# Weight operands split straight into the slot of a pair, their stores moved, attention blocks respaced

## The reference

```
attn:  q, k, v of (4, 8, 576, 64), cut into chunks of 64 rows;
       softmax(q_c k_c^T / 8) v_c inside each chunk  ->  x of 2304 tokens x 512
mlp 1: h = x @ w_in (512 x 2048);  g = h - tanh(h);               x = g @ w_out (2048 x 512)
mlp 2: h = x @ w_in (512 x 2048);  g = h * tanh(log(1 + exp(h))); out = g @ w_out
```

## Time and profile before

| | |
|---|---|
| device time, median of 2 | 1030.31 us (1028.92 to 1031.69) |
| the profiled execution, its device time | 1033.9 us |
| span from its first to its last instruction | 1032.1 us |
| PE busy | 860.1 us, 83% |
| DVE, ACT, POOL busy | 609.7, 381.0, 228.2 us |
| mean granted clock of TensorE | 0.907 |
| DMA | 180.48 MB, mean 175 GB/s |

### The profile page before, as it was taken

The page is one execution under the profiler, slowest core; times in us unless marked ns, Lnnn a source line. Parts: engine busy times, 40 slices in busy tenths (PEclk is TensorE's granted clock), DMA queues, the critical chain, the costliest instruction groups (busy, mean ns, idle before and its releaser), DMA issues.

```text
span 1032.1 us, 13626 instructions
## 1 busy us (share of the span) xinstructions
PE 860.1 (83%) x5298; PEld 782.0 (76%) x5298; DVE 609.7 (59%) x871; ACT 381.0 (37%) x539; POOL 228.2 (22%) x325
## 2 busy tenths in 40 slices
PE   8978667498547677998767666999999999999998
PEld 7977666498546566887666666898898988898986
DVE  6754445276324444663454443788888777787776
ACT  4432332142222222432233323455455344454453
POOL 4221433331222333323453432011110000000000
PEclk9988878799878788998888887999999999999999
DMA  7542456622435554444556587345396133752211
GB/s 249 180 137 89 144 165 220 209 79 104 171 147 181 203 200 167 153 154 174 203 214 214 214 318 273 119 157 198 140 385 234 74 143 120 309 204 102 113 72 62
DMA packets 51456, 180.48 MB, mean 175 GB/s; under 512 B 8768, under 2 KB 12608, under 8 KB 51392
## 3 DMA queue, kind: packets, MB, share of 16 engines
q1 hardware_dynamic: 33696, 112.74, 30.1%
q0 software_dynamic: 17696, 66.86, 18.4%
HBM read 125.04 MB, written 50.59 MB: 170 GB/s over the span
## 4 chain that ended last, share of the span: by engine, by line
PE 45%; DMA 10%; DVE 6%; POOL 4%; ACT 3%; issue 1%; ACTq 0%; DVEq 0%
PE psum L1473 6%; PE psum L1474 6%; PE psum L1472 6%; PE psum L1454 6%; PE psum L1455 6%; PE psum L1453 6%; DMA t_lo<-o_lo 5%; DMA s_lo<-o_lo 4%; DVE o_lo L934 2%; ACT o_hi L656 2%; PE psum L1337 2%; PE psum L1356 1%; PE psum L1338 1%; PE psum L1339 1%; PE psum L1357 1%
## 5 line engine op out<-in xcount | busy, mean ns | idle before, releaser
L934 DVE TENSOR_TENSOR o_lo<-pool_words,o_hi 128x768 fp32r<-128x768 f32 (+1 forms) x54 | 47.0, 870 | 116.2 <-ACT o_hi L656 116.2
L1454 PE MATMUL psum<-w_lo,w_hi 128*128 128x384 f32 x288 | 97.6, 339 | 0.0
L656 ACT ACTIVATE o_hi<-pool_words 128x768 fp32r<-128x768 f32 (+1 forms) x54 | 41.7, 772 | 150.9 <-DMA t_lo<-o_lo 74.0
L1455 PE MATMUL psum<-w_hi,w_lo 128*128 128x384 f32 x288 | 97.0, 337 | 0.0
L1453 PE MATMUL psum<-w_hi 128*128 128x384 f32 x288 | 96.3, 335 | 0.7 <-DVE pool_words L1111 0.7
L1337 PE MATMUL psum<-x_hi,w_hi 128*128 128x384 f32 x32 | 17.5, 548 | 94.0 <-DVE pool_words L1005 93.9
L1278 PE MATMUL psum<-g_hi,w_hi 128*128 128x384 f32 x128 | 50.1, 391 | 44.2 <-DMA pool_words<-pool_words 44.2
L1337 PEld LDWEIGHTS psum<-x_hi,w_hi 128*128 128x128 f32 x32 | 9.2, 286 | 96.8 <-issue 96.8
L1337 PE MATMUL psum<-w_hi 128*128 128x384 f32 x192 | 66.5, 346 | 15.4 <-DVE pool_words L994 13.1
L1474 PE MATMUL psum<-w_hi,g_lo 128*128 128x512 f32 x192 | 76.1, 396 | 0.0
L1473 PE MATMUL psum<-w_lo,g_hi 128*128 128x512 f32 x192 | 75.9, 395 | 0.0
(11 more groups left out here) (171 smaller groups left out, 2395.3 us busy)
## 6 DMA issues: line engine op xcount, KB each, us to landing
w_hi<-s_hi SPq DMA_DIRECT2D x40, 896.0 KB, 5.5
w_lo<-s_lo SPq DMA_DIRECT2D x40, 896.0 KB, 7.8
pool_words<-w POOLq DMA_DIRECT2D x32, 256.0 KB, 3.7
pool_words<-w_out POOLq DMA_DIRECT2D x32, 256.0 KB, 5.5
t_hi<-o_hi POOLq DMA_DIRECT2D x21, 384.0 KB, 3.5
t_lo<-o_lo POOLq DMA_DIRECT2D x21, 384.0 KB, 5.3
w_hi<-t_hi SPq DMA_DIRECT2D x18, 384.0 KB, 5.5
w_lo<-t_lo SPq DMA_DIRECT2D x18, 384.0 KB, 7.3
```

What stands on the lines that cost most here:

```text
L656: act.activation(step_halves(k)[0], step_source(k), ACT.Copy).then_inc(step_hi_done, 1)
L934: dve.tensor_tensor(lo, step_source(k), hi.bitcast(f32), ALU.subtract).then_inc(step_lo_done, 1)
L1454: pe.matmul(ps, a_hi, t_lo_words[:, k, :], start=False, stop=False, skip_group_check=i in (M5, M3))
L1455: mm = pe.matmul(ps, a_lo, t_hi_words[:, k, :], start=False, stop=end, skip_group_check=i in (M5, M3))
```

## The change

1. Weight operands of `w1` ("direct" steps) are split straight into the slot of their pair: no buffer, no store before use, and no `load_slot` for the first wide group. PE's `product1` waits for the split's parts. `keep_slot`, by SP, writes a finished slot to DRAM for the second wide group; `load_slot` is left for pairs 8 to 15 and the second MLP.
2. The other steps are spread anew: w2's operands 0 and 1, w1's 0 and 1 and two token steps in group 1 of the plain stage (none in group 0), w1's 2 to 7 beside pairs 1 to 6, w2's 2 to 7 beside pairs 8 to 14, the second token set beside pairs 9 to 15.
3. From w2's operand 3 on, `STEP_BUFFER` alternates between buffer 0 and a new buffer 2 (the second weight step stays in 1), and a third raw buffer holds every other operand.
4. Steps of pair 8 and later are stored by SP (`by_sync`), the rest by POOL; on POOL the stores now stand ahead of the sums.
5. Blocks 3 to 11 are respaced; `keep_x(t)` waits for `shift(t + 1)` and stands behind the exp; `shift` no longer waits for `keep_x`.
6. Two of the four last `y1` steps of the plain groups move ahead of pair 0; three token-operand splits (`x1_hi`, `x1_lo`) and block 12's normalisation move with them.

```diff
-TOKEN_STEPS = (M1, M5, M3, M7, M6, M2, M4)
+TOKEN_STEPS = (M1, M2, M5, M3, M7, M6, M4)
-BLOCK_AT = {(0, 5): 3, (0, 8): 4, (0, 11): 5, (0, 14): 6, (1, 1): 7, (1, 4): 8, (1, 7): 9, (1, 9): 10, (1, 11): 11}
+BLOCK_AT = {(0, 6): 3, (0, 10): 4, (0, 14): 5, (1, 1): 6, (1, 4): 7, (1, 7): 8, (1, 9): 9, (1, 12): 10, (1, 14): 11}
...
+_T = [[("tokens", s, i) for i in range(7)] for s in range(SUPERS)]
+_G1 = [(f, parts("weights", 0)[f - 1]) for f in (1, 2, 3)]
+_G1 += [(5, ("direct", 0, 0)), (6, _T[0][0]), (6, ("direct", 0, 1)), (7, ("direct", 0, 2))]
+_G1 += [(8, ("direct", 1, 0)), (8, _T[0][1]), (9, ("direct", 1, 1)), (10, ("direct", 1, 2))]
+_G1 += [(f, parts("weights", 1)[f - 10]) for f in (10, 11, 12)]
+place_steps([("group", f) for f, _ in _G1], [step for _, step in _G1])
+for _q in range(1, PAIRS - 1):
+    _d = parts("direct", _q + 1)
+    if _q == 2:
+        place_steps([(_q, 0)], _T[0][3:4])
+    place_steps([(_q, 1)], _d[0:1])
+    if _q in (1, 3, 4):
+        place_steps([(_q, 2)], [_T[0][{1: 2, 3: 5, 4: 6}[_q]]])
+    place_steps([(_q, 3), (_q, "w1")], _d[1:3])
+    if _q == 2:
+        place_steps([(_q, "w1")], _T[0][4:5])
+place_steps([(PAIRS, 3), (PAIRS + 1, 1), (PAIRS + 1, 2), (PAIRS + 1, 3)], parts("weights", 2)[0:2] + [_T[1][0], ("weights", 2, 2)])
+for _i in range(1, 6):
+    _w = parts("weights", 2 + _i)
+    place_steps([(PAIRS + 1 + _i, r) for r in range(4)], [_w[0], _T[1][_i], _w[1], _w[2]])
+place_steps([(2 * PAIRS - 1, 0)], _T[1][6:7])
...
+RAW_BUFFER = [1, 0, 1, 0] + [0] * 6 + [0, 2, 0, 2, 0, 2]
+    elif STEP_INDEX["weights", 3, 0] <= _k < EARLY_STEPS:
+        STEP_BUFFER.append(2 if next(b for b in reversed(STEP_BUFFER) if b in (0, 2)) == 0 else 0)
...
+def by_sync(k):
+    return k < EARLY_STEPS and STEP_PAIR[k] != "group" and STEP_PAIR[k] >= PAIRS
...
+            def behind_step(k):
                 what, n, i = STEPS[k]
                 pool.wait_ge(step_lo_done, k + 1)
+                if what != "direct" and not by_sync(k):
+                    to_hi, to_lo = step_target(k)
+                    from_hi, from_lo = step_halves(k)
+                    pool.dma_start(to_hi, from_hi.bitcast(f32)).then_inc(step_stored[STEP_BUFFER[k]], 16)
+                    pool.dma_start(to_lo, from_lo.bitcast(f32)).then_inc(step_stored[STEP_BUFFER[k]], 16)
+                if what == "tokens" and i + 1 < len(TOKEN_STEPS) and not (n == 0 and i == 1):
+                    add_tokens(n, i + 1)
+                if what != "tokens" and i == 0:
+                    add_weights(JOBS.index((what, n)))
...
+            def keep_slot(q):
+                r = q % 2
+                at = r * 7 * BLOCK
+                sp.wait_ge(step_lo_done, STEP_INDEX["direct", q, 2] + 1)
+                sp.dma_start(s_hi[q], w_hi[:, 0, at:at + 7 * BLOCK].bitcast(f32)).then_inc(slot_kept[r], 16)
+                sp.dma_start(s_lo[q], w_lo[:, 0, at:at + 7 * BLOCK].bitcast(f32)).then_inc(slot_kept[r], 16)
...
             for q in range(PAIRS1):
+                for k in range(EARLY_STEPS):
+                    if by_sync(k) and STEP_PAIR[k] == q:
+                        store_step(k)
...
+                if 2 <= q + 1 < PAIRS:
+                    keep_slot(q + 1)
+                if q + 2 >= PAIRS:
+                    load_slot(q + 2)
                 if t + 1 < TILES:
                     order_blocks(t + 1)
...
             def keep_x(t):
                 if t < TILES - 1:
-                    act.wait_ge(scores_ready, t + 2)
+                    act.wait_ge(shifted, t + 2)
...
+                if what == "direct" and i == 0:
+                    if n < 2:
+                        act.wait_ge(h_ready, FT - (-(n + 1) * 7 * BLOCK // D_MODEL))
+                    else:
+                        act.wait_ge(product1_ready, 7 * (n - 1))
+                        act.wait_ge(slot_kept[n % 2], 32 * (n // 2))
...
             def product1(q, place):
-                pe.wait_ge(slot_loaded[r], 32 * (q // 2 + 1))
+                if w == 0:
+                    pe.wait_ge(step_lo_done, STEP_INDEX["direct", q, max(0, (WEIGHT_OF[i] - 1) // 2)] + 1)
+                else:
+                    pe.wait_ge(slot_loaded[r], 32 * (q // 2 - PAIRS // 2 + 1))
```

More of the change, by code:

```diff
@@ L108 @@
-LAST_TOKEN_STEP = {s: STEPS.index(("tokens", s, 6)) for s in range(SUPERS)}
-STEP_BUFFER = [1 if what == "weights" and i == 1 and n > 0 else 0 for what, n, i in STEPS]
-RAW_BUFFER = [1, 0, 1, 0, 1] + [0] * 11
+STEP_INDEX = {step: _k for _k, step in enumerate(STEPS)}
+LAST_TOKEN_STEP = {s: STEP_INDEX["tokens", s, 6] for s in range(SUPERS)}
+JOBS = [step[0:2] for step in STEPS if step[0] != "tokens" and step[2] == 0]
+RAW_BUFFER = [1, 0, 1, 0] + [0] * 6 + [0, 2, 0, 2, 0, 2]
+STEP_BUFFER = []
+for _k, (_what, _n, _i) in enumerate(STEPS):
+    if _what == "direct":
+        STEP_BUFFER.append(None)
+    elif _what == "weights" and _i == 1:
+        STEP_BUFFER.append(1)
+    elif STEP_INDEX["weights", 3, 0] <= _k < EARLY_STEPS:
+        STEP_BUFFER.append(2 if next(b for b in reversed(STEP_BUFFER) if b in (0, 2)) == 0 else 0)
+    else:
+        STEP_BUFFER.append(0)
@@ L254, in step_source @@
             at, size = RAW_PARTS[i]
-            return raw[RAW_BUFFER[n]][:, at:at + size]
+            return raw[RAW_BUFFER[JOBS.index((what, n))]][:, at:at + size]
         def step_halves(k):
             what, n, i = STEPS[k]
+            if what == "direct":
+                at, size = WEIGHT_PARTS[i]
+                at += n % 2 * 7 * BLOCK
+                return [part[:, 0, at:at + size] for part in (w_hi, w_lo)]
             halves = o_hi[STEP_BUFFER[k]], o_lo[STEP_BUFFER[k]]
@@ L262, in step_halves, with step_target @@
             return [o[:, 0:WEIGHT_PARTS[i][1]] for o in halves]
+        def step_target(k):
+            what, n, i = STEPS[k]
+            if what == "tokens":
+                return [t[n, TOKEN_STEPS[i]].rearrange("p (k n) -> p k n", k=HALF_K) for t in (t_hi, t_lo)]
+            at, size = WEIGHT_PARTS[i]
+            return [part[PAIRS + n, :, at:at + size] for part in (s_hi, s_lo)]
         psum = ctx.enter_context(nc.psum_tensor("psum", [P, 8, 512], f32))
@@ L434, in _ @@
                     load_w2_out(1)
-                store_step(k)
-                if k == 1:
-                    load_raw(1)
-                if what == "weights" and i == 2:
-                    behind = [n for n in range(j + 1, 2 * PAIRS) if RAW_BUFFER[n] == RAW_BUFFER[j]]
-                    if behind:
-                        load_raw(behind[0])
+                    load_raw(JOBS.index(("weights", 3)))
+                behind_step(k)
                 q = STEP_PAIR[k]
-                if STEP_AT.get((q, 3)) == k:
+                if k + 1 == EARLY_STEPS or STEP_PAIR[k + 1] != q:
                     for r in ("w0", "w1"):
@@ L451, in _ @@
                 if pair in LATE_STEP_AT:
[L452 removed]
+                    behind_step(LATE_STEP_AT[pair])
         @block.sync
@@ L674, in mlp1_group @@
                         split_chunk_hi(f + 2)
-                    if ("group", g, f) in STEP_AT:
-                        step_hi(STEP_AT["group", g, f])
-                    if g == 1 and f >= FT - 3:
-                        for place in ((0, 1), (2, 3), (4,))[f - FT + 3]:
-                            x1_hi(0, place)
+                    for k in STEP_AT.get(("group", f), ()) if g == 1 else ():
+                        step_hi(k)
+                split_g_hi(FT * g + FT - 1)
                 if g == 0:
-                    split_g_hi(FT - 1)
                     tanh(FT)
@@ L759, in _ @@
                 mlp1_group(g)
-            x1_hi(0, 5)
+            for place in (2, 3, 4):
+                x1_hi(0, place)
             for q in range(PAIRS1):
@@ L956, in mlp1_group @@
                         split_chunk_lo(f + 2)
-                    if ("group", g, f) in STEP_AT:
-                        step_lo(STEP_AT["group", g, f])
-                    if g == 1 and f >= FT - 3:
-                        for place in ((0, 1), (2, 3), (4,))[f - FT + 3]:
-                            x1_lo(0, place)
+                    for k in STEP_AT.get(("group", f), ()) if g == 1 else ():
+                        step_lo(k)
+                split_g_lo(FT * g + FT - 1)
                 if g == 0:
-                    split_g_lo(FT - 1)
                     minus_tanh(FT)
@@ L1068, in _ @@
                 mlp1_group(g)
-            x1_lo(0, 5)
+            for place in (2, 3, 4):
+                x1_lo(0, place)
+            normalise(12)
+            turn_blocks(12)
             for q in range(PAIRS1):
```

200 lines of the change are left out of this document (101 added, 99 removed).

## The result

The changed kernel takes 901.4 us in the median of its runs (898.5 to 904.2) against 1030.3 before: a ratio of 0.8749, interval 0.862 to 0.8877. The profiled execution has a span of 896.8 us at a mean granted clock of 0.975, against 1032.1 at 0.907. The same kernel, measured again beside the last three experiments, took 904.7 us with a span of 902.0.

The account below looks back on a forecast made before the run. Store chains through one buffer were taken to bound the pairs, block-ordering waits the plain stage. Gains of 26 + 2.5 + 7.5 + 33 + 1.5 + 38 + 11 = 119.5 us took 1030.3 to 911, stated as 912, range 892 to 950.

Parts of the forecast that it names:

- pair 0: First pair after the plain stage: seven products and two y1 steps, 15 us against 17.7, a gain of 2.5.
- The stall put at 3.3 us: Plain stage: PE's wait for a block three steps f after the last, 2.7 to 4.1 us, three times.
- the two put at 7.3: Plain stage: PE's waits for blocks two steps f after the last, 6.9 to 8.3 us, twice.
- Half clock was put at 13: Plain stage: PE time lost to the lowered clock, 13 us instead of 22, with six stalls instead of ten.
- 13.0 + 8 + 2: Pairs 2 to 6, block cycle: scores to transposes, ordering issue and landing, values and scores; 23 us, 23.5 with half clock.
- the stall that I put at 1 to 2 us a pair: Pairs 10 to 14: stall from late output weights and the first step's store, making 17.7 us a pair, bounds 16.0 and 21.
- Two of the signs of being wrong: Listed: third weight step waits over 2 us for a store; DVE subtractions lengthen beside POOL; PE waits for `keep_slot` or late split.
- The first, a chain of stores in a new place: Pairs 10 to 15: third weight step waits for the first one's store, 21.5 us a pair, 935 in all; chance 0.11.
- The second, exclusion throughout: DVE and POOL exclude each other, 4.8 us a pair; pairs 10 to 14 take 20.5, 936 in all; chance 0.11.
- The third, the block chain not shorter: Plain-stage waits stay at 4 and 9 us, the cycle beside pairs at 26; 934 us in all; chance 0.11.
- The fifth, that the chains stay as they are: Buffers or places leave the store chains unchanged, only the plain stage gains; 1000 us in all; chance 0.01.
- The fourth, a split waiting for the slot's keep: Pairs 3 to 6: ACT's direct split waits for the slot's store, 25 us each if landing exceeds 50; 1040 us; chance 0.02.

Follow-up runs that it names:

- old blocks: The changed kernel with blocks 3 to 11 ordered at their old steps f: 916.2 us, ratio 0.8886.
- diagonal: The changed kernel with four of a block's eight ordering DMAs replaced by four copies on ACT: 885.4 us, ratio 0.8576.
- one buffer: The changed kernel without its third step buffer, all but each second weight step sharing buffer 0, SP still storing: 932.4 us, ratio 0.9033.
- thin sums: The changed kernel with POOL's sums for w1's operands and the first super's tokens only 8 columns wide, output incomplete: 909.5 us.
- the last three experiments: On the changed kernel: ACT copies for half the block ordering plus later PE block waits, 874.1 us; POOL sums 8 columns wide, 909.5; all of these, 864.9.

## Why the prediction was right

The two limits that were named, a chain of stores and a chain of block work that more of PE's work has to cover, are what the experiments show, so the mechanism was right, and the time with it. Most terms were too small: their sum was 119.5 us, the spans differ by 135.3. Each term against its stretch:

| stretch | forecast gain | measured |
|---|---|---|
| plain stage | 26 | 28.8 |
| pair 0 | 2.5 | -1.2 |
| pair 1 | 7.5 | 9.1 |
| pairs 2 to 6 | 33 | 36.2 |
| pair 9 | 1.5 | 3.3 |
| pairs 10 to 14 | 38 | 45.1 |
| pair 15 | 11 | 14.7 |
| second MLP | 0 | -0.7 |

*Plain stage.* Waits of 29 us in six stalls were forecast, 30.2 in six came, and none in group 0. The sum is better than its parts. The stall put at 3.3 us was 9.1 at block 7, whose words landed 9.3 us after the transposes; the two others of that kind were 1.8 and 2.6, the two put at 7.3 were 5.9 and 7.0, that across the seam 3.9 for 4.5. That these cancel is luck. Half clock was put at 13, and PE's busy time of 149.3 over the 140.6 of work makes it 9. `old blocks` shows that spacing gives 15 to 19 of the 28.8 us, not all of them. One small term fell: `keep_x` was to take 0.7 us off the chain, but scores to transposes went from 6.33 to 6.11.

*Pair 0* was wrong in sign: 15.2 us were forecast, 18.9 came. I had priced its products and y1 steps at full clock and block 12's chain, which does end inside it. What I didn't price is the split of the next x at its start, which `add_x` on POOL feeds. The timeline of pair 0:

```profile
200.19 5.41 DVE L977 TENSOR_TENSOR w_lo<-pool_words,w_hi 128x768 fp32r<-128x768 f32 x3 [0.50 <-ACT w_hi L675]
...
202.29 2.49 POOL L445 TENSOR_TENSOR pool_words<-pool_words 128x768 f32<-128x768 f32 x1 [0.90 <-DVE w_lo L977]
...
209.51 0.41 PE L1419 MATMUL psum<-w_hi 128*128 128x384 f32 x1 [2.51 <-DVE w_lo L977]
```

Three DVE instructions of 0.96 us take 5.41 beside POOL's sums, and PE waits 2.5 us in one place for such a split (1.4 more in two others, for which the profile names no releaser), at a clock of 0.91. It is the new spacing that brings them here. In `old blocks` the same three take 5.44 us, but start 2.3 us ahead of the pair's first product instead of 0.5 us behind it, and pair 0 takes 14.6 us, as forecast.

*Pairs 2 to 6.* I said that the block's chain would be what is left: 13.0 + 8 + 2. So it is beside pairs 4 to 6: 12.9 to the transposes, 6.2 to 7.4 to land, and values at the landing, a cycle of 20.4 to 21.5 us for the forecast's 23.5. Landing was mis-sized by 1 to 2 us. Beside pair 3 the cycle is 25.4: block 14's transposes come 16.5 us after its scores, behind DVE instructions grown long beside POOL (the longest stands below). That the stretch came so near is again in part a balance. And the gap that I said would be left in front of the values is 1.3 us in three waits; PE's largest wait in these pairs is still that for the fifth sum, 8.6 us in five, since DVE's list and the block's chain are about as long, as `diagonal` shows. That a landing can be 2 us late from one kernel to the next is a term that I didn't have.

*Pairs 10 to 14* hold the largest miss, 7 us: the stall that I put at 1 to 2 us a pair is 0.3 (81.5 / 5 - 16.0). I had charged the first step's store with 3.4 us and a busy queue, and the output weights with a late landing in every pair. The stores are no faster than that: in pairs 11 to 14, with the slot load ahead of it, the hi half took 3.1 to 3.9 us from issue to landing and the lo half 3.6 to 6.0. But only pair 13 (17.6 us) pays. There ACT waits 4.3 us for the output weights and 2.1 for the store, and PE 1.3. The four others take 15.9 to 16.2. The DMAs issued from 401.7 to 483.2 us (KB each, median us to landing):

```profile
w_hi<-s_hi SPq DMA_DIRECT2D x5, 896.0 KB, 6.6
w_lo<-s_lo SPq DMA_DIRECT2D x5, 896.0 KB, 9.1
...
s_hi<-o_hi SPq DMA_DIRECT2D x2, 384.0 KB, 3.5
s_lo<-o_lo SPq DMA_DIRECT2D x2, 384.0 KB, 4.8
```

*Pair 15.* Forecast 19.5, measured 16.0, its lower bound; a DMA share of 0.96 did it no harm. Nothing was tried on pairs 1, 9 and 15 by themselves, so the surplus of each (1.6, 1.8 and 3.7 us) stays without a shown cause.

*The signs.* Place 6's waits fell under 25 us (13.3), pairs 10 to 14 under 18 with a DMA share over 0.75. The period of pairs 3 to 6 was not 23 to 24 us but 19.9 to 23.4, the gap stayed at the fifth sum, and the clock was 0.86 in pair 9. Two of the signs of being wrong appeared, and both were small: DVE's subtractions grew long beside POOL, and ACT's third weight step waited over 2 us for a store, once, in pair 13:

```profile
461.18 0.63 ACT L733 ACTIVATE o_hi<-pool_words 128x512 fp32r<-128x512 f32 x1 [2.06 <-DMA s_lo<-o_lo]
```

*The rivals.* The first, a chain of stores in a new place, didn't come; `one buffer` shows the case in which it does, with pairs of 21.6 us for the 21.5 that it was given and 932 us for 935 (though its 4 us in pair 15 didn't come). The second, exclusion throughout, is there in part. The sharpest case:

```profile
254.46 3.98 DVE L1051 TENSOR_TENSOR g_lo<-pool_words,g_hi 128x768 fp32r<-128x768 f32 x1 [0.45 <-ACT g_hi L786]
...
254.63 0.56 POOL L403 DMA_DIRECT2D t_hi<-o_hi  x1
...
255.18 0.56 POOL L404 DMA_DIRECT2D t_lo<-o_lo  x1
...
255.75 1.86 POOL L427 TENSOR_TENSOR pool_words<-pool_words 128x768 f32<-128x768 f32 x1
```

An instruction of 0.96 us took 3.98, until 0.8 us after POOL's sum had ended. The Trainium skill ("SBUF — State Buffer", who interferes with whom) has the two exclude each other for the whole instruction, and the trace agrees that one ends only behind the other. It began 1.3 us before POOL's sum, though, and should by its own length have ended first; two issues of stores by POOL lie in between, and no experiment tells whether they held it. Up to the second MLP such excess (over 0.3 us above the median of the kind) is 19.3 us in 21 cases, 11.2 in 10 before. In pairs 10 to 14 it is 4.3 us in four cases, where the rival asked for up to 4.8 us a pair. In pairs 2 to 6 it is 6.3 us in five cases, nearly all in pairs 2 and 3, and there it costs: with thin sums pair 2 falls from 22.7 to 17.5 us. The third, the block chain not shorter, is half true: the chain is nearly as long as before, what grew is what covers it. The fifth, that the chains stay as they are, is out with place 6's waits. The fourth, a split waiting for the slot's keep, had its price decided at a landing of 50 us. It takes 5.1 and 6.5, and no wait of ACT for it stands in the trace.

## What to carry over

When a step must be stored before its buffer is free, the pair is as long as the chain of stores; a second buffer and another issuer for the stores each cure much of it, so price them together and test them apart. A chain that can't be shortened can still be given more work to hide it, and every microsecond of it that is then cut counts only until the next list is due. Giving a helper less to do can make the kernel slower, as `thin sums` did by 5 us: it releases its own transfers earlier, and the question is what they then run into.

## What I hadn't expected of the hardware

- For small transfers it seems to matter when others come more than how much they move. Eight DMAs of 32 KB landed 6.2 us after the transposes at best. In all 43 blocks with a raw load of three DMAs issued within 3.7 us of the start of their issue they landed 7.5 to 9.6 us after, with it at 4.4 us 6.2 to 8.8. Twice 896 KB of other traffic a pair cost at most 1 us a pair. Which of the coinciding things delays them was not tested.
- Issuing the eight takes 5.0 us, 0.6 each, and four take 2.4. The issue, not the bytes, is most of the landing of 6.2 us.
- Stores of 384 KB on SP's queue behind a slot load of 2 x 896 KB landed in 3.1 to 6.0 us at a DMA share of 0.86 and 318 GB/s; PE lost 1.3 us in one pair of five, in which ACT also waited 4.3 us for the output weights.
- A DVE instruction that began 1.3 us before a sum of POOL still ended 0.8 us behind it, 3.98 us long instead of 0.96.
- At a DMA share of 0.96 (pair 15, 357 GB/s) PE still had 16.0 us of 16.0 busy.
- The granted clock was 1.00, the 2.4 GHz level, in the pairs whose PE had next to no gaps (10 to 15, and 7 and 8 as before), and was 0.86 to 0.97 in the stages where stalls were left. Before, it was 0.78 to 0.87 in pairs 1 to 6 and 9 to 15 and in the plain stage, and 1.00 in pair 0, which is 0.91 now.
